# One operand's low part moved to VectorE, PSUM banks handed back singly, and another layout of the last stores, in a fused attention and two-layer kernel

## The chip, the core and the metric

The kernel runs on one core of a Trainium2 chip. Five engines work beside each other, each through its own queue of instructions in order: TensorE (PE, with its weight loads shown as PEld), VectorE (DVE), ScalarE (ACT), GpSimd (POOL) and SyncE (SP), which here only issues DMAs. Engines wait for one another by semaphores. The metric is the time of the kernel on the device, in microseconds (us), median of several runs.

## The reference, cut to what matters

```python
kv = np.einsum('bhsd,bhse->bhde', k, v)            # (4, 8, 64, 64), sum over 576 positions
out = np.einsum('bhsd,bhde->bhse', q, kv)
out = out / np.sqrt(np.mean(out * out, axis=-1, keepdims=True) + 1e-06) * g_norm
x = out.transpose(0, 2, 1, 3).reshape(2304, 512)
h = x @ w_in                                       # layer 1: 512 -> 2048 -> 512
x = (h * (1.0 / (1.0 + np.exp(-h)))) @ w_out
a, b = x @ w_a, x @ w_b                            # layer 2: 512 -> 1536 -> 512
return (a * b) @ w_out2                            # (2304, 512) float32
```

## The kernel before, in words

**Stages.** The 2304 tokens are split into two groups (G = 0 and 1) of 1152, each of two batch rows. After the attention of group 0, the projections run in four segments: layer 1 of group 0, layer 1 of group 1, layer 2 of group 0, layer 2 of group 1 (`SEGS`, numbered 0 to 3, with `PAIR0` = 0, 8, 16, 22, 28). A segment is cut into pairs of 128 hidden columns (8, 8, 6 and 6 of them); the attention of group 1 is done in small pieces between the steps of the first pairs (`attend`, with the steps listed in `KV_AT`, `Q_AT` and so on).

**Products.** Each up projection of a pair is a Strassen scheme of seven products (steps 0 to 6, `step` and `half`, matmuls at L777; L794 for the first two pairs). Every fp32 number is held as a high and a low fp32r part, and each product is made of three: high by high, high by low, low by high. The activations' low parts are `x_lo[:, n]`, one for each of the seven operands, and are made once at the start of a segment: ACT rounds (`x_round`, L1111), then DVE or POOL subtracts (`x_rest`, L1404 for DVE, L634 for POOL). `DVE_RESTS` and `POOL_RESTS` (L87, L88) say which does which, and PE waits for the count that `x_split` gives. In segments 1 to 3 POOL makes the one of operand 6: at the end of `up(u)` (L536 to L558) of the segment's first product. There it stands ahead of the weights of the next product, which POOL also splits (L523, L525).

**Down projections.** The tiles of a pair's down projection are computed one pair later between the steps, by `down1` (L863 to L865, layer 1) and `down2` (L885 to L887, layer 2), in two PSUM banks in turn, BANK_D and BANK_D + 1 (`tile_bank`, from a count of turns). DVE adds each finished tile to `xy` (`flush1` L1473, `flush2` L1484), and `wait_turn` makes PE wait until a bank's last reader is done.

**Keys and values.** `kv(G, h)` (L709) writes both of these banks, and ACT copies the result to `kv_sb` with four copies of 64x64, two for each bank (`kv_keep`, L1077). Both banks are then free at one count, `kv_kept` (L713). For group 1, four such products are made, at the steps in `KV_AT` = (0, 8, 17, 27). Behind the last three stand the rest of a step, of six matmuls, and then a tile of `down1`.

**DVE's queue in layer 2.** The order is written out by hand. In the first pair of segment 2 (`layer2_after_1`, L1608) it is: late_rest 5, flush 3 and 4, `add(ua, 1)`, flush 5. In the other pairs (`layer2`, L1641) it is: late_rest 5, `add(ua, 0)`, flush2 2, `add(ua, 1)`. `add` (L1427) joins two halves of the Strassen sums; PE may begin step 6 only behind `add(ua, 1)` (`may_begin`, L804).

**The end.** After the last pair nine tiles of 128 tokens remain. DVE flushes each, and each is stored by two DMAs, one on SP's queue for the lower 64 partitions and one on ACT's for the upper 64 (`half_tile`; L502, L1310). The ninth is computed and stored in two halves of 256 columns, so as four quarters (`last_down` L899 to L901, `last_flush` L1492, `last_quarter`; L505, L1313). The banks of its halves are those of `last_bank`: the tile's own and the other one of the pair, which tile 8 (j = 7) holds until its flush. The program ends when `stored` has its full count.

Of the kernel before, what the change touches and what calls it, by code (L numbers as in the profile page):

```python
# [15 lines left out]
def fused_attention_ffn_kernel(nc, q, k, v, g_norm, w_in, w_out, w_a, w_b, w_out2, out):  # L16
    BATCH, HEADS, SEQ, HD = q.shape
    D, FF1 = w_in.shape
    FF2 = w_a.shape[1]
    HALF = P // 2  # L20
# [63 lines left out]


    FIRST_ROUNDS = ((0, 0), (7, 0), (0, 1), (7, 1), (3, 0), (6, 0), (3, 1), (6, 1), (5,), (1,), (2,), (4,))
    POOL_RESTS = (((0, 0), (0, 1), (7, 0), (7, 1), (5, 0), (5, 1)), (6,))  # L87
    DVE_RESTS = (((3, 0), (6, 0), (3, 1), (6, 1), (1, 0), (1, 1), (2, 0), (2, 1), (4, 0), (4, 1)),  # L88
                 (0, 1, 2, 3, 4, 5))


    PIECES = [(c, slice(s * PART, (s + 1) * PART)) for c in range(2) for s in range(2)]
# [6 lines left out]
    with ExitStack() as ctx:  # L99
        def sem(name):  # L100
            return ctx.enter_context(nc.semaphore(name))
# [68 lines left out]
        kv_mm = sem("kv_mm")  # L170
        q_ready = sem("q_ready")
        kv_kept = sem("kv_kept")
        kv_kept2 = sem("kv_kept2")
        qT_mm = sem("qT_mm")
        qT_kept = sem("qT_kept")
# [144 lines left out]
            dst = out[(2 * G + m) * SEQ:(2 * G + m + 1) * SEQ].rearrange("(p t) d -> p t d", t=ROWS)[:, n, :]  # L320
            return dst, xy[:, G, :].rearrange("p (j d) -> p j d", d=D)[half * HALF:(half + 1) * HALF, j, :]

        def last_quarter(half, c):

            dst, src = half_tile(GROUPS - 1, TOK_TILES - 1, half)
            cols = slice(c * (D // 2), (c + 1) * (D // 2))
            return dst[:, cols], src[:, cols]

        def staged(G, h):

# [4 lines left out]
            return [(h, j) for h in range(PAIRS) for j in range(JS) if steps[h][j] == at]  # L335


        unit_turn, tile_turn, turns = {}, [], 0
        for pp in range(PAIR0[-1] + 1):
            tiles = D_TILES[SEGS[seg_of(pp - 1)][1]] if pp else 0  # L340
            steps = len(PLAIN[0]) if pp == 1 else STEPS if pp < PAIR0[1] else 0
            for n in range(steps):
                if n < STEPS:
                    at = STEPS * pp + n
                    turns += 2 * KV_AT.count(at)
                    for kind in (RESULT_AT, Q_AT, PROD_AT):
                        for unit in units(at, kind):
                            unit_turn[kind, unit] = turns
                            turns += 1
                for _ in range(0 if pp == 0 else PLAIN_TILES_AFTER[n] if pp == 1 else TILES_AFTER[n]):  # L350
                    tile_turn.append(turns)
                    turns += 1
            for _ in range(tiles if steps == 0 else 0):
                tile_turn.append(turns)
                turns += 1
# [3 lines left out]

        def last_bank(c):  # L360

            return BANK_D + (tile_turn[DOWN0[-1] - 1] + c) % 2

        def unit_bank(kind, h, j):
            return BANK_D + unit_turn[kind, (h, j)] % 2
# [31 lines left out]

        def x_split(seg, n, c=1):

            kind, what = (1, n) if seg else (0, (n, c))  # L400
            if what in POOL_RESTS[kind]:
                at = POOL_RESTS[kind].index(what) + 1
                return side_ready, at + (len(POOL_RESTS[0]) + (seg - 1) * len(POOL_RESTS[1]) if seg else 0)
            at = DVE_RESTS[kind].index(what) + 1
            return x_ready, at + (len(DVE_RESTS[0]) + (seg - 1) * len(DVE_RESTS[1]) if seg else 0)

        def temps(seg):

# [21 lines left out]
        @block.sync  # L430
        def _(sp):
            def raw_free(r):

                n = max(n for n in range(len(SEGS)) if RAW0[n] <= r)
                layer = SEGS[n][1]
                p, what = divmod(r - RAW0[n], layer + 1)
                if what == layer:
                    sp.wait_ge(d_ready, 2 * (PAIR0[n] + p + 1))
                elif p < PLAIN_PAIRS and n == 0:
                    sp.wait_ge(w_ready, RING * (p + 1))  # L440
                else:
                    sp.wait_ge(w_sum, sums_before(PROD0[n] + layer * p + what + 1, 4))

            def load_raw(r):
                n = max(n for n in range(len(SEGS)) if RAW0[n] <= r)
                layer = SEGS[n][1]
                p, what = divmod(r - RAW0[n], layer + 1)
                if r >= RAWS:
                    raw_free(r - RAWS)
                dst = raw[:, r % RAWS, :]  # L450
                cols = slice(2 * p * P, 2 * (p + 1) * P)
                if what == layer:
                    w = w_out if layer == 1 else w_out2
                    dst, src = dst.rearrange("p (f n) -> p f n", f=2), w[cols, :].rearrange("(f p) n -> p f n", p=P)
                else:
                    w = w_in if layer == 1 else (w_a, w_b)[what]
                    dst = dst.rearrange("p (c n) -> p c n", c=KT)
                    src = w.rearrange("(c p) n -> p c n", p=P)[:, :, cols]
                sp.dma_start(dst, src).then_inc(raw_in[r % RAWS], 16)

            def load_heads(h):


                before = PAIRS + h - 1 if h else 0
                sp.wait_ge(kv_mm, before + 1)
                sp.wait_ge(qT_mm, JS * (before + 1))
                for which in range(2):
                    sp.dma_start(*heads(1, h, which)).then_inc(kv_in[0], 16)
                for bb in range(2):
                    for odd in range(2):  # L470
                        sp.dma_start(*head_by_tiles(h, bb, odd)).then_inc(q_in[0], 16)


            for h in range(PAIRS):
                sp.dma_start(*heads(0, h, 0)).then_inc(kv_in[h], 16)
                sp.dma_start(*queries(h, 0)).then_inc(q_in[h], 16)
                if h == 1:
                    for half in range(2):
                        sp.dma_start(gcol[half * HALF:(half + 1) * HALF, 0:1],
                                     g_norm.rearrange("(p a) -> p a", a=1)).then_inc(g_in, 16)  # L480
            sp.dma_start(*raw_half(0)).then_inc(raw_in[0], 16)

            sp.wait_ge(q_in[PAIRS - 1], 32)
            load_heads(0)
            load_raw(1)
            for r in range(2, RAW0[-1]):
                load_raw(r)
                if r == 2:
                    load_heads(1)
                if r == 5:  # L490
                    load_heads(2)
                if r == 8:
                    load_heads(3)
                if r == RAW0[3] + 5:
                    sp.wait_ge(flushed, DOWN0[3])
                    for j in range(TOK_TILES):
                        for half in range(2):
                            sp.dma_start(*half_tile(0, j, half)).then_inc(stored, 16)

            for j in range(TOK_TILES - 1):  # L500
                sp.wait_ge(flushed, down0(PAIR0[-1] - 1) + j + 1)
                sp.dma_start(*half_tile(1, j, 0)).then_inc(stored, 16)  # L502
            for c in range(2):
                sp.wait_ge(flushed, DOWN0[-1] + c)
                sp.dma_start(*last_quarter(0, c)).then_inc(stored, 16)  # L505
            sp.wait_ge(stored, 16 * (2 * GROUPS * TOK_TILES + 2))

        @block.gpsimd
        def _(pool):
# [26 lines left out]
            def up(u):  # L536
# [17 lines left out]
                nc.gpsimd.tensor_tensor(t0, b21, t1, ALU.subtract).then_inc(w_sum, 1)  # L554
                pool.wait_ge(w_sum, done + 4)
                ready(u, 6, t0)
                if u == PROD0[seg_of(pair_of(u))]:
                    x_rest(seg_of(pair_of(u)), 6)  # L558

            def second_up():  # L560

# [125 lines left out]
        def _(pe):  # L687
# [7 lines left out]
            def kv(G, h):  # L695
# [15 lines left out]
                                           start=(t == 0), stop=(t == ROWS - 1))  # L711
                mm.then_inc(kv_mm, 1)
                turn[b0] = turn[b1] = (kv_kept, PAIRS * G + h + 1)  # L713

            def q_turn(G, h, j, bank):
                i = UNITS * G + JS * h + j
# [317 lines left out]
        def _(act):  # L1034
# [30 lines left out]
            def kv_keep(G, h):  # L1065
# [2 lines left out]
                if n >= 2:  # L1068
                    act.wait_ge(o_mm, JS * (n - 1))
                act.wait_ge(cleared, 2)  # L1070
                for odd, bank in enumerate((BANK_D, BANK_D + 1)):
                    if n == 0 and odd:

                        continue
                    rows = slice(odd * HALF, odd * HALF + HD)
                    for bb in range(2):
                        cp = nc.scalar.copy(kv_sb[rows, h % 2, bb, rows], ps[bb * HALF:(bb + 1) * HALF, bank, 0:HD])  # L1077
                cp.then_inc(kv_kept, 1)

            def qT_keep(G, h, j, bank):  # L1080
# [224 lines left out]
                else:  # L1305
                    layer2(pp)
            g_round(PAIR0[-1] - 1, 3)
            for j in range(TOK_TILES - 1):
                act.wait_ge(flushed, down0(PAIR0[-1] - 1) + j + 1)
                nc.scalar.dma_start(*half_tile(1, j, 1)).then_inc(stored, 16)  # L1310
            for c in range(2):
                act.wait_ge(flushed, DOWN0[-1] + c)
                nc.scalar.dma_start(*last_quarter(1, c)).then_inc(stored, 16)  # L1313

        @block.vector
        def _(dve):
# [291 lines left out]
            def layer2_after_1(pp):  # L1608
# [12 lines left out]
                add(ua, 0, halves(held[:, 0, :]))  # L1621
                late_rest(pp, 5)
                flush(3, 4)
                add(ua, 1, halves(held[:, 2, :]))
                flush(5, 5)
                add(ua, 2, halves(held[:, 3, :]))
# [14 lines left out]
            def layer2(pp):  # L1641
# [4 lines left out]
                flush2(pp - 1, 1)  # L1646
                late_rest(pp, 5)
                add(ua, 0, halves(held[:, 0, :]))
                flush2(pp - 1, 2)
                add(ua, 1, halves(held[:, 2, :]))  # L1650
                flush2(pp - 1, 3)
# [83 lines left out]
```

## Time and profile before

| what | value |
|---|---|
| median of 3 runs | 870.26 us (870.24 to 873.62) |
| the profiled execution | 873.04 us, span 871.2 us |
| PE busy | 860.4 us, 99% of the span |
| PEld, DVE, ACT, POOL busy | 93%, 59%, 32%, 70% |
| granted TensorE clock | 0.998 |
| moved by DMA | 55.56 MB, mean 64 GB/s |

The span is what the trace covers, from the first instruction of the program to the last. Times in the trace count from its start. The page lists busy time by engine, the chain of work that ended last, and groups of instructions. In a timeline a row may stand for several equal instructions (x2); its length runs from the first's start to the last's end, and matmuls overlap in their pipeline, so their starts tell more than their lengths. Idle time before an instruction stands in brackets with what ended it.

### The profile page before, as it was taken

Reading aid. Unit: us, or ns where it says so; the run is one execution under the profiler, and the core shown is the slowest. Engines: PE = TensorE matmul, PEld = TensorE weight load, DVE = VectorE, ACT = ScalarE, POOL = GpSimd, SP = SyncE. Lnnn points to the kernel's source line nnn. Section 1 sums busy time; section 2 is a strip of 40 time slices with the busy share of each in tenths; the row PEclk is TensorE's granted clock in tenths of the full one; section 3 lists DMA queues with packets and bytes.
Section 4 is the critical chain, followed back from the end, with each engine's and each line's share of the span. In section 5 each row is a group of like instructions: output and inputs, shape, how many; then the busy total and the mean of one; then the engine's idle time right before and its main releaser. Section 6 shows DMA issues by size and latency. Waiting matters only on the chain.

```text
span 871.2 us, 16097 instructions
## 1 busy us (share of the span) xinstructions
PE 860.4 (99%) x6208; PEld 813.8 (93%) x6208; DVE 510.6 (59%) x776; ACT 279.0 (32%) x465; POOL 610.1 (70%) x889
## 2 busy tenths in 40 slices
PE   8899999999999999999999999999999999999998
PEld 5699999999999999999999999999999999999997
DVE  4665656757886666665765355364484553544636
ACT  3764434534543323222532122121242211212210
POOL 2566545666578777766778697797889876877760
PEclk9999999999999999999999999999999999999999
DMA  9664123111011111111101111021011330210104
GB/s 300 158 156 106 49 57 75 50 49 49 26 49 49 46 28 50 50 49 49 49 25 49 50 49 49 25 63 60 25 49 49 109 98 25 74 49 25 49 25 109
DMA packets 47002, 55.56 MB, mean 64 GB/s; under 512 B 11728, under 2 KB 32464, under 8 KB 46928
## 3 DMA queue, kind: packets, MB, share of 16 engines
q1 hardware_dynamic: 44192, 49.55, 19.9%
q10 hardware_dynamic: 2736, 4.98, 1.8%
q8 instruction: 51, 0.84, 0.4%
q14 instruction: 23, 0.19, 0.1%
HBM read 49.81 MB, written 4.72 MB: 63 GB/s over the span
## 4 chain that ended last, share of the span: by engine, by line
PE 98%; DVE 1%; issue 1%; ACT 0%; POOL 0%; POOLq 0%
PE ps L777 49%; PE ps L863 8%; PE ps L864 8%; PE ps L865 8%; PE ps L885 6%; PE ps L887 6%; PE ps L886 6%; PE ps L794 3%; PE ps L737 2%; PE ps L747 1%; PE ps L989 1%; PE ps L709 1%; PE ps L723 1%; DVE o_sb L1350 0%; DVE stat L1331 0%
## 5 line engine op out<-in xcount | busy, mean ns | idle before, releaser
L777 PE MATMUL ps<-x_hi,w_hi 128*128 128x288 f32 x1064 | 229.8, 297 | 0.5 <-issue 0.3
L777 PE MATMUL ps<-x_lo,w_hi 128*128 128x288 f32 x1064 | 228.1, 296 | 0.0
L777 PE MATMUL ps<-x_hi,w_lo 128*128 128x288 f32 x1064 | 226.8, 295 | 0.0
L777 PEld LDWEIGHTS ps<-x_hi,w_hi 128*128 128x128 f32 x1064 | 179.0, 188 | 13.7 <-issue 5.1
L777 PEld LDWEIGHTS ps<-x_hi,w_lo 128*128 128x128 f32 x1064 | 171.7, 189 | 0.0
L777 PEld LDWEIGHTS ps<-x_lo,w_hi 128*128 128x128 f32 x1064 | 169.9, 188 | 0.0
L1142 ACT COPY kept<-ps 128x576 f32<-128x576 f32 x114 | 73.2, 642 | 288.1 <-PE ps L777 287.6
L523 POOL TENSOR_SCALAR w_hi<-wt 128x256 fp32r<-128x256 f32 x152 | 69.9, 460 | 123.4 <-PE ps L777 116.4
L1473 DVE TENSOR_TENSOR xy<-xy,ps 128x384 f32<-128x384 f32 (+1 forms) x188 | 94.0, 510 | 89.0 <-PE ps L865 88.7
L863 PE MATMUL ps<-g_hi,d_hi 128*128 128x384 f32 x384 | 129.0, 336 | 0.2
L864 PE MATMUL ps<-g_lo,d_hi 128*128 128x384 f32 x384 | 128.9, 336 | 0.0
L865 PE MATMUL ps<-g_hi,d_lo 128*128 128x384 f32 x384 | 128.6, 335 | 0.0
L525 POOL TENSOR_TENSOR w_lo<-wt,w_hi 128x256 fp32r<-128x256 f32 x152 | 114.9, 756 | 12.7
L1484 DVE TENSOR_TENSOR xy<-xy,ps 128x512 f32<-128x512 f32 x89 | 61.0, 685 | 94.2 <-PE ps L887 94.2
L525 POOL TENSOR_TENSOR w_lo<-raw,w_hi 128x256 fp32r<-128x256 f32 x122 | 92.8, 761 | 10.2
L523 POOL TENSOR_SCALAR w_hi<-raw 128x256 fp32r<-128x256 f32 x122 | 52.4, 430 | 57.2 <-PE ps L777 54.2
L885 PE MATMUL ps<-d_hi,g_hi 128*128 128x512 f32 x214 | 84.5, 395 | 0.0
L1167 ACT CAST g_hi<-ps 128x576 fp32r<-128x576 f32 x86 | 55.3, 644 | 89.6 <-DVE ps L1433 54.4
L887 PE MATMUL ps<-d_hi,g_lo 128*128 128x512 f32 x214 | 83.8, 392 | 0.0
L886 PE MATMUL ps<-d_lo,g_hi 128*128 128x512 f32 x214 | 83.6, 391 | 0.0
L1427 DVE TENSOR_TENSOR held<-kept,ps 128x576 f32<-128x576 f32 x62 | 46.8, 755 | 55.6 <-PE ps L777 55.6
L672 POOL TENSOR_TENSOR d_lo<-raw,d_hi 128x512 fp32r<-128x512 f32 x56 | 75.6, 1371 | 0.0
(111 smaller groups left out, 1236.7 us busy)
## 6 DMA issues: line engine op xcount, KB each, us to landing
raw<-in_moe_w_out_dram SPq DMA_DIRECT2D x28, 512.0 KB, 3.6
raw<-in_moe_w_in_dram SPq DMA_DIRECT2D x15, 512.0 KB, 3.5
raw<-in_moe_w_a_dram SPq DMA_DIRECT2D x12, 512.0 KB, 3.5
raw<-in_moe_w_b_dram SPq DMA_DIRECT2D x12, 512.0 KB, 3.5
kvq<-in_k_dram SPq DMA_DIRECT2D x8, 576.0 KB, 5.5
out_dram<-xy SPq DMA_DIRECT2D x26, 128.0 KB, 2.4
kvq<-in_v_dram ACTq DMA_DIRECT2D x4, 576.0 KB, 11.4
kvq<-in_v_dram SPq DMA_DIRECT2D x4, 576.0 KB, 5.9
```

The costliest lines, as they stand in the source:

```text
L523: nc.gpsimd.tensor_scalar(w_hi[:, slot], src, 1.0, 0.0, ALU.mult, ALU.add).then_inc(w_high, 1)
L525: nc.gpsimd.tensor_tensor(w_lo[:, slot], src, w_hi[:, slot].bitcast(F32), ALU.subtract).then_inc(w_ready, 1)
L672: nc.gpsimd.tensor_tensor(d_lo[:, pp % 2, f, :], w[:, f, :], d_hi[:, pp % 2, f, :].bitcast(F32), ALU.subtract).then_inc(d_ready, 1)
L777: mm = pe.matmul(ps[:, bank + s, 0:PART], w, x[:, n, c, s * PART:(s + 1) * PART], start=(begins and first), stop=last, skip_group_check=no ...
L863: pe.matmul(dst, hi, of_high, start=(f == 0), stop=False)
L864: pe.matmul(dst, hi, of_low, start=False, stop=False)
L865: mm = pe.matmul(dst, lo, of_high, start=False, stop=(f == 1))
L885: pe.matmul(dst, hi, d_hi[:, pp % 2, f, :], start=(f == 0), stop=False)
L886: pe.matmul(dst, hi, d_lo[:, pp % 2, f, :], start=False, stop=False)
L887: mm = pe.matmul(dst, lo, d_hi[:, pp % 2, f, :], start=False, stop=(f == 1))
L1142: nc.scalar.copy(halves(kept[:, n, :]), both(BANK_A)).then_inc(part_kept, 1)
L1473: op = nc.vector.tensor_tensor(dst, dst, src, ALU.add)
```

## The change

Four things are changed.

1. The low part of operand 6 in segments 2 and 3 is made by DVE, no more by POOL. In `layer2_after_1` it stands between flush 4 and `add(ua, 1)`, in `layer2` between `add(ua, 0)` and flush2 2. Segment 1 keeps it on POOL.
2. For the keys and values of group 1, a new semaphore `kv_first` is raised after ACT's two copies of the bank whose turn comes first; `kv_order` names it, and `kv_keep` copies it first. The other bank is freed by `kv_kept` as before.
3. The second half of the last tile goes to BANK_A (`last_bank`).
4. The last two tiles are stored over all 128 partitions (`last_tile`): tile j = 7 by one DMA on SP's queue, tile j = 8 by two DMAs of 256 columns each, the first on ACT's queue and the second on SP's. The DRAM side of these is indexed by 2 rows, 64 tokens and the columns; the SBUF side by 128 partitions and the columns.

```diff
-    POOL_RESTS = (((0, 0), (0, 1), (7, 0), (7, 1), (5, 0), (5, 1)), (6,))
+    POOL_RESTS = (((0, 0), (0, 1), (7, 0), (7, 1), (5, 0), (5, 1)), (6,), (), ())
     DVE_RESTS = (((3, 0), (6, 0), (3, 1), (6, 1), (1, 0), (1, 1), (2, 0), (2, 1), (4, 0), (4, 1)),
-                 (0, 1, 2, 3, 4, 5))
+                 (0, 1, 2, 3, 4, 5), (0, 1, 2, 3, 4, 5, 6), (0, 1, 2, 3, 4, 5, 6))
...
-        def last_quarter(half, c):
-
-            dst, src = half_tile(GROUPS - 1, TOK_TILES - 1, half)
-            cols = slice(c * (D // 2), (c + 1) * (D // 2))
-            return dst[:, cols], src[:, cols]
+        def last_tile(j, cols):
+
+
+            n = 2 * j - ROWS
+            dst = out[(2 * GROUPS - 1) * SEQ:].rearrange("(p t) d -> t p d", t=ROWS)[n:n + 2, :, cols]
+            return dst, xy[:, GROUPS - 1, :].rearrange("p (j d) -> p j d", d=D)[:, j, cols]
...
-            return BANK_D + (tile_turn[DOWN0[-1] - 1] + c) % 2
+            return (tile_bank(DOWN0[-1] - 1), BANK_A)[c]
+
+        def kv_order(G, h):
+
+            return (kv_turn[h] % 2, 1 - kv_turn[h] % 2) if G else (0, 1)
...
-            for j in range(TOK_TILES - 1):
+
+            for j in range(TOK_TILES - 2):
                 sp.wait_ge(flushed, down0(PAIR0[-1] - 1) + j + 1)
                 sp.dma_start(*half_tile(1, j, 0)).then_inc(stored, 16)
-            for c in range(2):
-                sp.wait_ge(flushed, DOWN0[-1] + c)
-                sp.dma_start(*last_quarter(0, c)).then_inc(stored, 16)
-            sp.wait_ge(stored, 16 * (2 * GROUPS * TOK_TILES + 2))
+            sp.wait_ge(flushed, DOWN0[-1] - 1)
+            sp.dma_start(*last_tile(TOK_TILES - 2, slice(0, D))).then_inc(stored, 16)
+            sp.wait_ge(flushed, DOWN0[-1] + 1)
+            sp.dma_start(*last_tile(TOK_TILES - 1, slice(D // 2, D))).then_inc(stored, 16)
+            sp.wait_ge(stored, 16 * (2 * TOK_TILES + 2 * (TOK_TILES - 2) + 3))
...
-                if u == PROD0[seg_of(pair_of(u))]:
-                    x_rest(seg_of(pair_of(u)), 6)
+                if u == PROD0[1]:
+                    x_rest(1, 6)
...
                 turn[b0] = turn[b1] = (kv_kept, PAIRS * G + h + 1)
+                if G:
+                    turn[BANK_D + kv_order(G, h)[0]] = (kv_first, h + 1)
...
-                for odd, bank in enumerate((BANK_D, BANK_D + 1)):
+                for place, odd in enumerate(kv_order(G, h)):
...
                     for bb in range(2):
-                        cp = nc.scalar.copy(kv_sb[rows, h % 2, bb, rows], ps[bb * HALF:(bb + 1) * HALF, bank, 0:HD])
+                        cp = nc.scalar.copy(kv_sb[rows, h % 2, bb, rows],
+                                            ps[bb * HALF:(bb + 1) * HALF, BANK_D + odd, 0:HD])
+                    if G and place == 0:
+                        cp.then_inc(kv_first, 1)
                 cp.then_inc(kv_kept, 1)
...
-            for j in range(TOK_TILES - 1):
+            for j in range(TOK_TILES - 2):
                 act.wait_ge(flushed, down0(PAIR0[-1] - 1) + j + 1)
                 nc.scalar.dma_start(*half_tile(1, j, 1)).then_inc(stored, 16)
-            for c in range(2):
-                act.wait_ge(flushed, DOWN0[-1] + c)
-                nc.scalar.dma_start(*last_quarter(1, c)).then_inc(stored, 16)
+            act.wait_ge(flushed, DOWN0[-1])
+            nc.scalar.dma_start(*last_tile(TOK_TILES - 1, slice(0, D // 2))).then_inc(stored, 16)
...
                 flush(3, 4)
+                late_rest(pp, 6)
                 add(ua, 1, halves(held[:, 2, :]))
...
                 add(ua, 0, halves(held[:, 0, :]))
+                late_rest(pp, 6)
                 flush2(pp - 1, 2)
```

## Rows read from the trace of the kernel before

**Rows 1.** The page: busy time by engine, chain that ended last, one group.

```profile
PE 860.4 (99%) x6208; PEld 813.8 (93%) x6208; DVE 510.6 (59%) x776; ACT 279.0 (32%) x465; POOL 610.1 (70%) x889
PE 98%; DVE 1%; issue 1%; ACT 0%; POOL 0%; POOLq 0%
L863 PE MATMUL ps<-g_hi,d_hi 128*128 128x384 f32 x384 | 129.0, 336 | 0.2
```

**Rows 2.** Waits: who waited for what, us in total, times, longest.

```profile
PEld ps L863 <- issue: 0.9, 3, 0.3
PEld ps L777 <- POOL w_lo L525: 0.6, 2, 0.3
PEld ps L899 <- DVE xy L1484: 0.3, 1, 0.3
```

**Rows 3.** Timeline behind the last product of keys: start, length, engine, line, operation.

```profile
143.85 0.87 ACT L1077 COPY kv_sb<-ps 64x64 f32<-64x64 f32 x4 [1.73 <-PE ps L709]
144.34 0.42 PE L777 MATMUL ps<-x_hi,w_lo 128*128 128x288 f32 x2
144.86 0.42 PE L863 MATMUL ps<-g_hi,d_hi 128*128 128x384 f32 x1
```

**Rows 4.** Timeline, PE and POOL, first pair of segment 3.

```profile
658.67 3.10 POOL L637 TENSOR_TENSOR x_lo<-xy,x_hi 128x288 fp32r<-128x288 f32 x4
...
661.21 0.39 PE L887 MATMUL ps<-d_hi,g_lo 128*128 128x512 f32 x1
661.87 0.50 PE L777 MATMUL ps<-x_hi,w_hi 128*128 128x288 f32 x2 [0.27 <-issue]
663.26 0.43 PE L777 MATMUL ps<-x_hi,w_lo 128*128 128x288 f32 x2
663.70 0.53 PE L777 MATMUL ps<-x_hi,w_hi 128*128 128x288 f32 x2
```

**Rows 5.** Timeline, ACT and DVE, the same pair.

```profile
654.62 1.16 ACT L1111 CAST x_hi<-xy 128x1152 fp32r<-128x1152 f32 x1
...
655.69 0.75 DVE L1427 TENSOR_TENSOR held<-kept,ps 128x576 f32<-128x576 f32 x1
658.67 0.69 DVE L1484 TENSOR_TENSOR xy<-xy,ps 128x512 f32<-128x512 f32 x1 [2.23 <-PE ps L887]
```

**Rows 6.** Timeline, DVE and PEld, first pair of segment 2.

```profile
450.79 0.55 DVE L1473 TENSOR_TENSOR xy<-xy,ps 128x384 f32<-128x384 f32 x1 [0.67 <-PE ps L865]
452.39 0.75 DVE L1427 TENSOR_TENSOR held<-kept,ps 128x576 f32<-128x576 f32 x1 [1.04 <-PE ps L777]
...
453.26 0.30 PEld L777 LDWEIGHTS ps<-x_hi,w_hi 128*128 128x128 f32 x2 [0.18 <-issue]
```

**Rows 7.** Line L1406: duration ns min/median/max, first and last start.

```profile
L1406 DVE TENSOR_TENSOR x_lo<-xy,x_hi x6: 1347/1353/1383, 231.3 to 648.9; 128x1152 fp32r<-128x1152 f32 x6
```

**Rows 8.** Timeline of the end, DVE and SP's queue.

```profile
868.18 0.42 DVE L1492 TENSOR_TENSOR xy<-xy,ps 128x256 f32<-128x256 f32 x1 [0.62 <-PE ps L901]
...
857.79 9.82 SPq L502 DMA_DIRECT2D out_dram<-xy  x8
...
867.14 0.47 SPq L502 DMA_DIRECT2D out_dram<-xy  x1
```

**Rows 9.** DMA in 855:872, 855:868 (busy tenths of 40 slices) and 858:868.

```profile
DMA packets 1601, 2.38 MB, mean 140 GB/s; under 512 B 320, under 2 KB 576, under 8 KB 1600
...
DMA  0000000000009993987196909991798378953987
...
q1 hardware_dynamic: 555, 0.91, 43.9%
q10 hardware_dynamic: 550, 0.91, 23.9%
```

**Rows 10.** DMA in 868.5:871.2 (one queue) and 869.4:871.2 (busy tenths).

```profile
q10 hardware_dynamic: 243, 0.27, 30.6%
...
DMA  9986542648999888999783100000000000000000
```

More of the change, by code:

```diff
@@ L172, in fused_attention_ffn_kernel @@
         kv_kept = sem("kv_kept")
+        kv_first = sem("kv_first")
         kv_kept2 = sem("kv_kept2")
@@ L335, in units @@
             return [(h, j) for h in range(PAIRS) for j in range(JS) if steps[h][j] == at]
-        unit_turn, tile_turn, turns = {}, [], 0
+        unit_turn, tile_turn, kv_turn, turns = {}, [], [], 0
         for pp in range(PAIR0[-1] + 1):
@@ L344, in fused_attention_ffn_kernel @@
                     at = STEPS * pp + n
-                    turns += 2 * KV_AT.count(at)
+                    if at in KV_AT:
+                        kv_turn.append(turns)
+                        turns += 2
                     for kind in (RESULT_AT, Q_AT, PROD_AT):
@@ L398, in x_split @@
         def x_split(seg, n, c=1):
[L400 to L405, printed above, removed]
+            what = n if seg else (n, c)
+            split, signal = (POOL_RESTS, side_ready) if what in POOL_RESTS[seg] else (DVE_RESTS, x_ready)
+            return signal, split[seg].index(what) + 1 + sum(len(rests) for rests in split[:seg])
         def temps(seg):
```

## The prediction, made before the changed kernel was built or run

> **What bounds the kernel now.** The page comes first: PE is busy 99% of the span and makes up 98% of the chain that ended last, so only three things can move the time: idle moments of PE, PE's own work (which this change leaves as it is) and what follows PE's last matmul [rows 1]. The list of waits shows how short these moments are: three waits ahead of a `down1` tile (0.9 us in all), two for POOL's weights (0.6), one at the end for a flush (0.3) [rows 2]. Then I read the timeline around each place that the change touches, by the starts of matmuls. In steady work the two matmuls of a kind at L777 start 0.13 apart, so what exceeds this is lost. The end was read from DVE's last flush to the last bytes of the stores. The profiled span is 871.2 us and the median of the runs 870.26; I work out a difference on the span and add it to the median.
>
> **Banks of keys and values.** Behind the last product of keys, the pair of matmuls at 144.34 should be followed by the `down1` tile at 144.34 + 2 x 0.13 = 144.60, and it starts at 144.86, when ACT has made its four copies (143.85 + 0.87 = 144.72) [rows 3]. Lost: 0.26, and another 0.08 because the first matmul after the stop runs 0.42 against a mean of 0.336 [rows 1, 3]. With the bank given back after two copies it is free at about 143.85 + 0.44 = 144.29, before PE wants it. The second bank is wanted a tile later, over 1 us behind, when all four copies are long done. The list of waits has three such stops, of 0.3 each on the load side [rows 2]; the other two lie behind the products at about 61 and 102 us. I take 3 x 0.32 = **-0.97 us** (between -0.7 and -1.0). The fourth product, with other work behind it, has none.
>
> **Operand 6 in segment 3.** POOL's subtraction takes 3.10 us, until 661.77, and PE's step 6 begins at 661.87, where it should have begun at 661.21 + 0.23 = 661.44: 0.43 lost [rows 4]. POOL then comes late with the next product's weights, and PE starts it at 663.70 where 663.26 + 0.26 = 663.52 was due: 0.18 lost, the stop put down to `w_lo` [rows 2, 4]. After the two stops the first pair of matmuls is longer by 0.08 and 0.10 (0.50 and 0.53 against 0.42 to 0.43) [rows 4]. Sum 0.79. On DVE the same subtraction of an operand in `xy` takes 1.35 us in all six cases, never over 1.38 [rows 7]. DVE is free for it: x_hi is there at 655.78, `add(ua, 0)` ends at 656.44, and then DVE idles 2.23 us until the flush at 658.67 [rows 5]. So it is done at 657.8, nothing behind it in DVE's queue moves, and step 6 finds it over 3 us early. Next late there would be `add(ua, 1)`, which has no delay now. I take **-0.80 us**. If the cover of 2.23 us were gone, the flush and PE's bank behind it would come up to 1.35 later.
>
> **Operand 6 in segment 2.** No stop of PE goes here, for POOL's subtraction was early enough. DVE has less room: flush 4 ends at 451.34 and `add(ua, 1)` starts at 452.39, 1.04 us of idle for 1.35 of work [rows 6, 7]. So `add` comes about 0.3 later. PE waits for this very `add` before step 6; its load already idles 0.18 before that [rows 6], so there is no slack and the delay goes to PE in full. **+0.27 us** (from 0.1, if the two operations overlap at their ends, to 0.6, if POOL's traffic slows the subtraction).
>
> **The last bank.** PE stops 0.3 ahead of the last half tile for the flush of tile 8 [rows 2]. BANK_A has been free since the last pair's sums, so the stop goes and the last flush (868.18) comes 0.3 earlier [rows 8]. It counts only if this flush leads to what ends last.
>
> **The last stores.** Here I expect the change to lose. In the last 17 us 20 DMAs leave 320 packets under 512 B, 16 to each: every store so far was shared by 16 DMA engines, which each report once [rows 9]. In all of them both sides have 64 partitions or rows as their outermost dimension. The new ones have 128 partitions on one side, but on the DRAM side an outermost dimension of 2. If a DMA is dealt to the engines along the outermost dimension, only 2 engines can have a share, and each carries 64 rows. No row of before shows such a DMA, so this is bounded from both sides. From below: 16 engines as before, costing nothing. From above: two engines, all three DMAs on the same two. Their speed: in 858:868 one queue moved 0.91 MB in 23.9% of 16 engines' 10 us = 38.2 us, 23.8 GB/s for each busy engine; the other needed 43.9%, so 13.0 GB/s [rows 9]. With rows of 1 KB it was 0.27 MB in 30.6% of 43.2 us = 20.4 GB/s [rows 10]. Tile 8 of the nine is 0.262 MB, 0.131 for each engine: 5.5 us. Tile 9, in rows of 1 KB, as much: 6.4 us. Tile 8's store is issued at 867.14 as before [rows 8]; the first bytes follow an issue by 1.1 us (issue at 857.79, traffic from the thirteenth slice, 858.9) [rows 8, 9]. So the last bytes come at 868.25 + 11.9 = 880.15. Now they come at about 870.4, 0.8 before the end of the span [rows 10]. The end would be at 880.95, **+9.75 us**, and the 0.3 of the last bank isn't on the path.
>
> The Trainium skill, in the page DMA: Bandwidth & Descriptors, section Why a DMA increments its semaphore by 16 and not by 1, says this outright: the number of engines is the largest up to 16 that divides the slowest dimension of both sides, so 2 here, and the lowest-numbered ones. The trace agrees for 64 and 128; no row of it shows a smaller number. The same page speaks for the change in its Rules for kernel authors: two transfers to disjoint halves of the partitions share the same engines, and one over 128 partitions is to be used. By that rule alone the end would be no later than now; that is rival A.
>
> **Sum of the forecast:** -0.97 - 0.80 + 0.27 + 9.75 = +8.25 us on the span, and 870.26 + 8.25 = **878.5 us**.
>
> **Rivals.**
> *All engines share the new stores (A).* Then the last bytes follow the last flush as they do now, with 0.3 from the last bank: -0.97 - 0.80 + 0.27 - 0.3 = -1.8, 868.4 us, no measurable difference. For it: every DMA of the trace has its 16 reports, and the SBUF side still has 128 partitions along which to deal [rows 9]. Against it: both sides must be cut at the same rows, and the DRAM side is offered as 2 blocks of 64. The point of decision is the number of packets under 512 B that the last three stores leave: 48 in this case, about 6 in the forecast. It ends on the other side of the forecast.
> *Two engines at the slower speed (C).* If the two disturb each other as the two queues did, 13.0 GB/s gives 0.262 MB / 13.0 = 20.2 us for each engine, and +18.05 in place of +9.75: 886.8 us. Against it: with two busy engines of 16 there is little to contend for, and most packets should be as fast as the better queue's.
> *The change does not remove the stops (D).* With all engines, but with new waits in the place of the old: a second release on ACT that comes as late as the first, or the 0.27 in segment 2 grown to 1.35 by a flush that is late too. About 870 us, same. Against it are the 0.3 us of room that two copies leave and DVE's 2.23 us of idle [rows 3, 5].
>
> **How the numbers follow.** Forecast 0.63, A 0.25, C 0.05, D 0.05, and 0.02 for A with a gain that I have missed. A measurement of this kernel can tell some 0.5%, 4.35 us, from no change. Slower by more is forecast and C: 0.68. Within it A and D: 0.30. Faster 0.02. The forecast's own range is 876.5 to 881.5: from 23.8 GB/s for both tiles (11.0 us) and first bytes 0.5 sooner, to 18 GB/s for both, midway to the slower queue (14.6 us). As cases on both sides hold most of the chance, the range of 8 in 10 must reach to A: 868.0 to 881.0 us, which leaves out C, the top of the forecast's own range and little else.
>
> **What would show it.** Right: PE's last matmul about 1.8 us earlier than now, near 866; no idle time before the three `down1` tiles; step 6 of segment 3 starting 0.23 behind the matmul before it; in segment 2 a `PEld` idle of about 0.45 in place of 0.18. The last DMAs take over 6 us from issue to landing, DMA is busy at 1 tenth for some 11 us with two engines, and of the packets under 512 B some 230 remain (14 x 16 + 3 x 2). Wrong: the last bytes within 2 us of the last flush, or 272 such packets (17 x 16). If PE ends later than now, the parts on DVE or on ACT were wrong.

## The result and the profile after

The changed kernel took 880.72 us (median of 4 runs, 879.26 to 881.22), the kernel before beside it 870.25 us. The ratio is 1.0106 with a 95% interval of 1.0085 to 1.0127: slower by 7.4 to 11.1 us. The profiled execution took 880.93 us, with a span of 878.9 us.

| | before | after |
|---|---|---|
| median | 870.25 us | 880.72 us |
| span of the profiled execution | 871.2 us | 878.9 us |
| start of PE's last matmul | 867.86 us | 865.49 us |
| from there to the end of the span | 3.4 us | 13.4 us |

The last two rows hold the whole result. PE is done earlier, and what follows it takes four times as long. The page of the changed kernel, busy time by engine and the chain of work that ended last:

```profile
PE 858.8 (98%) x6208; PEld 813.6 (93%) x6208; DVE 513.8 (58%) x778; ACT 278.7 (32%) x465; POOL 605.9 (69%) x881
PE 95%; DMA 2%; DVE 1%; SPq 1%; issue 0%; ACT 0%; POOL 0%
```

PE's busy time fell by 1.6 us against [rows 1]. The 2% of DMA in the chain are not the stores but a load at the start, as the chain in order of time shows (start, length, what):

```profile
5.47 16.00 DMA kvq<-in_q_dram
```

The same 2% stand in the second profile of the kernel before, which has none of the change. This chain ends with DVE's last flush and leaves the stores out, so their price has to be read from the DMA rows.

**The end.** First the timeline of SP's and ACT's queues and of PE in the changed kernel, then its DMA in 867.4:879 (in the two rows of slices each is 0.29 us: busy tenths of the 16 engines, and GB/s), then the DMA packets in 855:879.

```profile
865.10 0.62 SPq L510 DMA_DIRECT2D out_dram<-xy  x1
866.26 0.53 SPq L512 DMA_DIRECT2D out_dram<-xy  x1
...
865.54 1.09 ACTq L1324 DMA_DIRECT2D out_dram<-xy  x1
...
865.49 0.28 PE L910 MATMUL ps<-d_hi,g_lo 128*128 128x256 f32 x1
...
DMA  0020111111111111111111111111111111111000
GB/s 7 35 21 21 35 56 42 56 42 53 56 46 53 49 46 53 49 46 60 42 49 56 46 46 46 49 49 49 49 49 46 46 49 49 49 46 46 7 0 0
...
DMA packets 1511, 2.38 MB, mean 99 GB/s; under 512 B 230, under 2 KB 486, under 8 KB 1510
```

Where [rows 9, 10] have most of the engines busy until 870.4, here one tenth of them (2 of 16) is busy for over 9 us, at 49 GB/s on the mean. The packets under 512 B are 230 = 14 x 16 + 3 x 2: two reports from each of the three new DMAs.

**Behind the keys.** The timeline of the changed kernel behind the last product of keys, as in [rows 3]:

```profile
142.15 0.88 ACT L1086 COPY kv_sb<-ps 64x64 f32<-64x64 f32 x4 [1.73 <-PE ps L716]
142.64 0.43 PE L786 MATMUL ps<-x_hi,w_lo 128*128 128x288 f32 x2
142.91 0.34 PE L872 MATMUL ps<-g_hi,d_hi 128*128 128x384 f32 x1
```

The tile starts at 142.91, 0.27 behind the pair before it, while ACT is still copying the other bank until 143.03. The stop is gone.

**Segment 3.** The end of the tile and the start of step 6, as in [rows 4]; then DVE's new operation with the flush behind it, as in [rows 5]:

```profile
659.92 0.39 PE L896 MATMUL ps<-d_hi,g_lo 128*128 128x512 f32 x1
660.15 0.42 PE L786 MATMUL ps<-x_hi,w_hi 128*128 128x288 f32 x2
...
655.07 1.57 DVE L1417 TENSOR_TENSOR x_lo<-xy,x_hi 128x1152 fp32r<-128x1152 f32 x1
657.38 0.69 DVE L1495 TENSOR_TENSOR xy<-xy,ps 128x512 f32<-128x512 f32 x1 [0.74 <-PE ps L896]
```

Step 6 follows after 0.23, without a stop, and DVE is done 0.74 us before the flush.

**Segment 2.** DVE, POOL and PEld around step 6 of the first pair, as in [rows 6]:

```profile
449.23 1.94 DVE L1417 TENSOR_TENSOR x_lo<-xy,x_hi 128x1152 fp32r<-128x1152 f32 x1
451.09 0.74 DVE L1438 TENSOR_TENSOR held<-kept,ps 128x576 f32<-128x576 f32 x1
...
449.22 0.73 POOL L532 TENSOR_TENSOR w_lo<-wt,w_hi 128x256 fp32r<-128x256 f32 x1
449.92 1.84 POOL L553 TENSOR_TENSOR wt<-raw 128x256 f32<-128x256 f32 x1
...
451.95 0.19 PEld L786 LDWEIGHTS ps<-x_hi,w_hi 128*128 128x128 f32 x1 [0.90 <-issue]
```

The idle time ahead of step 6 grew from 0.18 to 0.90 us. DVE's operation took 1.94 us and not 1.35, and POOL's beside it 1.84, where another of the same shape takes 0.74.

**Step by step on PE.** The same matmul can be found in both traces, since PE's order did not change. How much earlier it starts after the change:

| stretch (times of before) | earlier by | of which here |
|---|---|---|
| until 38 us, ahead of the projections | 1.05 us | 1.05 |
| tiles behind the keys at 64, 104, 145 us | 2.03 | 0.31 + 0.34 + 0.33 |
| step 6 of segment 2, 453 us | 1.29 | -0.74 |
| segment 3, 662 to 664 us | 2.03 | 0.75 |
| last half tile, 867 us | 2.37 | 0.33 |

The first row is not the change, as the second profile of the kernel before shows below. Without it PE is 1.3 us earlier at the end. The gains behind the keys, in segment 3 and at the last bank are read from these starts; they recur in three other kernels with the same parts, but no run takes one of them out alone.

### The profile page after: what moved, and what is told of

Same layout as the page of the kernel before. It is cut to its first block, busy times and chain, and to the rows that moved or that the text cites. A ratio compares the mean times of both kernels' runs of the same rounds, so it can differ in the third digit from the quotient of the medians.

```text
span 878.9 us, 16088 instructions
## 1 busy us (share of the span) xinstructions
PE 858.8 (98%) x6208; PEld 813.6 (93%) x6208; DVE 513.8 (58%) x778; ACT 278.7 (32%) x465; POOL 605.9 (69%) x881
## 4 chain that ended last, share of the span: by engine, by line
PE 95%; DMA 2%; DVE 1%; SPq 1%; issue 0%; ACT 0%; POOL 0%
PE ps L786 48%; PE ps L873 8%; PE ps L874 8%; PE ps L872 8%; PE ps L894 6%; PE ps L896 6%; PE ps L895 6%; PE ps L803 3%; DMA kvq<-in_q_dram 2%; PE ps L746 2%; PE ps L756 1%; PE ps L732 1%; PE ps L716 1%; DVE x_lo L1417 0%; SPq L480 0%
## 5 line engine op out<-in xcount | busy, mean ns | idle before, releaser
L532 POOL TENSOR_TENSOR w_lo<-raw,w_hi 128x256 fp32r<-128x256 f32 x122 | 93.6, 767 | 10.2
```

Of the source, the lines that this page charges most:

```text
L532: nc.gpsimd.tensor_tensor(w_lo[:, slot], src, w_hi[:, slot].bitcast(F32), ALU.subtract).then_inc(w_ready, 1)
```

## The experiments

Each is compared with the kernel before run on the same chip beside it, whose median was 871.5 to 871.7 us there.

### The changed kernel with the old stores

```diff
-            for j in range(TOK_TILES - 2):
+            for j in range(TOK_TILES - 1):
                 sp.wait_ge(flushed, down0(PAIR0[-1] - 1) + j + 1)
                 sp.dma_start(*half_tile(1, j, 0)).then_inc(stored, 16)
...
-            sp.dma_start(*last_tile(TOK_TILES - 2, slice(0, D))).then_inc(stored, 16)
...
+            for c in range(2):
+                sp.wait_ge(flushed, DOWN0[-1] + c)
+                sp.dma_start(*last_quarter(0, c)).then_inc(stored, 16)
...
```

> The changed kernel with the last stores of before (halves and quarters of 64 partitions each), all else as changed. Theory (two engines carry the new stores, and these are the whole loss): the gains that the two profiles show remain, 0.9 us behind the keys, 0.66 in segment 3, 0.3 at the last bank, against 0.64 lost in segment 2, so 1.2 us under the kernel before, about 869.0, with the last bytes within 2 us of the last flush. Rival (part of the loss is elsewhere, since the medians lie 10.5 us apart and the two spans only 7.7): still 0.5 to 3 us above the kernel before, 870.7 to 873.

Measured: ratio 0.9993 (0.9983 to 1.0002), median 870.07 us against 871.52 over 11 runs. The loss is gone with the stores; the rival is ruled out, if narrowly, for it wanted a kernel at least 0.5 us slower than before and the interval ends at +0.2. The ratio is worth 0.6 us, and the expected gain of 1.2 us lies just inside the other edge of the interval. The profile has all the steps of the table at nearly the same sizes (0.31, 0.33, 0.33, -0.70, 0.74, 0.32), but from PE's last matmul to the end it takes 3.7 us, 0.3 more than before. The timeline of this kernel's end shows why: DVE's last flush, and ACT's issue of the last quarter, with that issue in the kernel before behind them:

```profile
866.12 0.42 DVE L1502 TENSOR_TENSOR xy<-xy,ps 128x256 f32<-128x256 f32 x1 [0.30 <-PE ps L908]
...
866.83 0.62 ACTq L1323 DMA_DIRECT2D out_dram<-xy  x1
```

```profile
868.63 0.55 ACTq L1313 DMA_DIRECT2D out_dram<-xy  x1
```

The flush ends at 866.54, and the DMA is issued at 866.83: ACT's queue was still issuing the quarter before. In the kernel before, the issue followed the flush at once (868.60 and 868.63). So what BANK_A gave is taken back by the queue here, where each queue has a DMA for each half tile.

### The new stores alone

```diff
-            for j in range(TOK_TILES - 1):
+            for j in range(TOK_TILES - 2):
...
+            sp.dma_start(*last_tile(TOK_TILES - 2, slice(0, D))).then_inc(stored, 16)
+            sp.wait_ge(flushed, DOWN0[-1] + 1)
+            sp.dma_start(*last_tile(TOK_TILES - 1, slice(D // 2, D))).then_inc(stored, 16)
...
```

> The kernel before with nothing but the new stores of the last two tiles; the order of the banks, of keys and of operand 6 is that of before. Theory: the first bytes 1.1 us behind the issue at 867.1, then 11.3 to 11.9 us on two engines, the end 9.75 us (9.3 to 10.3) later than before, about 880 us, and PE's last matmul where it was. In the DMA rows of the end 230 packets under 512 B. Rival (the loss needs the other parts too, the earlier end of PE or the load of the queues): under +8 us.

Measured: ratio 1.0134 (1.0118 to 1.0149), median 882.21 us. The profile, with SP's issues and its DMA in 855:879.6 (slices of 0.615 us), has the forecast's shape:

```profile
865.75 0.62 SPq L505 DMA_DIRECT2D out_dram<-xy  x1
867.25 0.53 SPq L507 DMA_DIRECT2D out_dram<-xy  x1
...
DMA  0000969678594949596111111111111111111100
GB/s 0 0 0 0 193 233 200 227 153 270 117 270 127 217 150 206 197 203 227 40 20 23 23 43 53 52 50 50 50 50 50 50 48 48 48 48 47 48 33 0
```

From PE's last matmul to the end it takes 13.08 us against 3.39: +9.7, where +9.75 was expected. The interval of the ratio gives 10.3 to 13.0 us, so the timed runs lost at least 0.6 us more than the profiled one. Part of this lies in the start, as the section on the second profile shows: by their mean clock all four runs had the stretch of lower clock there, and the kernel before had it in only 10 of its 21; against these 10 the median lies 10.2 us higher. The rest stays unexplained. The rival (a smaller loss without the other parts) is out.

### One tile, and three tiles, on the new pattern

```diff
-            for j in range(TOK_TILES - 1):
+            for j in range(TOK_TILES - 2):
...
+            sp.wait_ge(flushed, DOWN0[-1] - 1)
+            sp.dma_start(*last_tile(TOK_TILES - 2, slice(0, D))).then_inc(stored, 16)
             for c in range(2):
                 sp.wait_ge(flushed, DOWN0[-1] + c)
                 sp.dma_start(*last_quarter(0, c)).then_inc(stored, 16)
```

> The kernel before, with tile j = 7 alone stored by one DMA over 128 partitions; the last tile in quarters as before. Theory (two engines at 24 GB/s each): 0.131 MB on each engine, 5.4 us from 868.25, with the quarters' rows on the same engines behind or between them: the end 3 to 4.5 us later than before, under half of the loss of both tiles. Rival (a fixed delay for such a DMA, whatever its size): 8 us or more, as with both tiles, or none where the quarters are alone at the end.

Measured: ratio 1.0049 (1.0031 to 1.0066), +2.7 to +5.8 us; in the profile the end lies 8.13 us behind PE's last matmul, +4.7, a little over the expected size. The DMA packets of this kernel in 855:884 are those of 18 plain stores and one on two engines (18 x 16 + 2 = 290):

```profile
DMA packets 1571, 2.38 MB, mean 82 GB/s; under 512 B 290, under 2 KB 546, under 8 KB 1570
```

The rival (a fixed delay of 8 us, or none) is out.

```diff
+            sp.wait_ge(flushed, DOWN0[-1] - 2)
+            sp.dma_start(*last_tile(TOK_TILES - 3, slice(0, D))).then_inc(stored, 16)
+            sp.wait_ge(flushed, DOWN0[-1] - 1)
+            sp.dma_start(*last_tile(TOK_TILES - 2, slice(0, D))).then_inc(stored, 16)
...
```

> The kernel before with three tiles (j = 6, 7 and 8) stored as the changed kernel stores two. Theory (all such DMAs queue on the same two engines, and their bytes set the end): one more tile of 0.262 MB is 5.5 us on the two engines, of which 1.36 us lie ahead of the issue of the next: the end 4.0 to 4.5 us later than with two tiles, some 14 us later than before, near 884.5 us. Rival (each DMA has two engines of its own): no later than with two tiles.

Measured: ratio 1.0146 (1.0127 to 1.0164), median 884.37 us. From PE's last matmul to the end it takes 17.0 us, 3.9 more than with two tiles and 13.6 more than before. The DMA of this kernel in 855:884 (slices of 0.725 us):

```profile
GB/s 0 82 268 170 204 178 198 201 178 229 172 226 76 37 42 23 34 45 51 54 51 51 45 51 51 51 51 51 51 51 48 51 48 48 49 49 14 0 0 0
DMA packets 1481, 2.38 MB, mean 82 GB/s; under 512 B 200, under 2 KB 456, under 8 KB 1480
```

Four such DMAs share the same 49 to 51 GB/s and leave 12 x 16 + 4 x 2 = 200 small packets. The loss thus goes by bytes (4.7, 9.7 and 13.6 us for one, two and three tiles), it is no fixed delay, and the DMAs don't get two engines each, which would give 98 GB/s.

### Rows that two divides and four does not

```diff
+        def rows_of(j, half):
+            dst, src = half_tile(1, j, half)
+            cut = 62 if j == TOK_TILES - 2 else HALF
+            return [(dst[a:b], src[a:b]) for a, b in ((0, cut), (cut, HALF)) if a < b]
...
-                sp.dma_start(*half_tile(1, j, 0)).then_inc(stored, 16)
+                for dst, src in rows_of(j, 0):
+                    sp.dma_start(dst, src).then_inc(stored, 16)
```

> The kernel before, with the two halves of tile j = 7 each stored as 62 partitions and then the last 2, so plain patterns of 62 x 512 and 2 x 512 on both sides. Theory (a DMA is shared by the largest number of engines up to 16 that divides the outermost counts): 2 engines for each of the four, 64 rows of 2 KB on each of the same two engines, 5.4 us, and the last quarters behind them: the end 3 to 4.5 us later than before, and 296 packets under 512 B in the last 17 us in place of 320. Rival (only the outermost dimension of 2 in the DRAM pattern confines it, plain rows are spread over all): at most 0.5 us later, and over 320 such packets.

Measured: ratio 1.0072 (1.0054 to 1.0091). The DMA packets in 855:884, and SP's queue:

```profile
DMA packets 1577, 2.38 MB, mean 82 GB/s; under 512 B 296, under 2 KB 552, under 8 KB 1576
...
867.77 2.54 SPq L512 DMA_DIRECT2D out_dram<-xy  x2
```

There are 296 small packets (18 x 16 + 4 x 2): the 62 rows of a plain pattern went to two engines as well. So it is a divisor of the outermost counts that decides, and not the form of the pattern with its block of 2. The Trainium skill states this rule in the page DMA: Bandwidth & Descriptors, section Why a DMA increments its semaphore by 16 and not by 1; the 230, 290, 200 and 296 packets agree with it. The runs have only the cases of 2 and 16 engines, so they can't tell the largest divisor up to 16 from the largest power of two.

The size was missed: from PE's last matmul to the end it takes 9.8 us, +6.4 where 3 to 4.5 was expected. The issue of the last two quarters on SP's queue took 2.54 us. The same two issues in the kernel before, and in the kernel with one tile on the new pattern:

```profile
867.65 1.44 SPq L505 DMA_DIRECT2D out_dram<-xy  x2
```

```profile
866.49 1.30 SPq L514 DMA_DIRECT2D out_dram<-xy  x2
```

With one tile on the new pattern two engines were loaded too, yet the issue was no longer than before. So a load on two engines is not enough to hold the issuing queue back; here both queues feed them, and each has one more DMA to issue. The two engines moved some 0.29 MB (the tile and their share of the quarters) between about 868.1 and 876.5, which is an estimate of 35 GB/s for both, against 49 before. Why this is slower wasn't settled.

### POOL held while DVE subtracts

```diff
                 if u == PROD0[1]:
                     x_rest(1, 6)
+                if u == PROD0[2]:
+                    pool.wait_ge(*x_split(2, 6))
```

> The changed kernel, with POOL held in the first pair of segment 2 until DVE has made the low part of operand 6. In the changed kernel this DVE operation took 1.94 us beside POOL's work, against 1.35 in six cases of the kernel before. Theory (DVE and POOL slow each other down where both work in SBUF): 1.35 to 1.40 us, and the stop ahead of step 6 falls from 0.78 to about 0.2 us. Rival (DVE is slowed by something else there, such as the traffic of a load, or the place in the queue): 1.9 us and 0.7 to 0.8 as before.

DVE's and PEld's timeline of this kernel, and POOL's wait:

```profile
450.27 1.35 DVE L1419 TENSOR_TENSOR x_lo<-xy,x_hi 128x1152 fp32r<-128x1152 f32 x1
...
452.40 0.30 PEld L788 LDWEIGHTS ps<-x_hi,w_hi 128*128 128x128 f32 x2 [0.32 <-issue]
...
451.70 0.74 POOL L547 TENSOR_TENSOR wt<-raw 128x256 f32<-128x256 f32 x1 [5.78 <-DVE x_lo L1419]
```

DVE takes 1.35 us again. By the starts of matmuls PE loses 0.20 us before step 6, as expected, where it lost 0.78 in the changed kernel and 0.06 in the kernel before. So POOL's work beside it had made the operation slow. The one run took 881.34 us and says nothing about the gain: the lower clock at its start lasted 6.8 us, twice as long as in the changed kernel.

The timeline of the changed kernel, above, fits turns taken: DVE starts at 449.23, just behind POOL's operation of 0.73 at 449.22, and 0.7 + 1.35 is about its 1.94; POOL's next, begun at 449.92, ends 0.6 behind DVE's. The Trainium skill describes this in the page SBUF — State Buffer, section SBUF: two separate sides: a DVE operation with two SBUF inputs and a GpSimd one that reads SBUF need the same pair of ports, and whichever starts first holds it for its whole length. The rows agree within 0.2 us.

The trace of the kernel before had already shown it, in the groups of the same line that [rows 7] leaves out:

```profile
L1406 DVE TENSOR_TENSOR x_lo<-kvq,x_hi x9: 1346/1550/2443, 234.9 to 651.5; 128x1152 fp32r<-128x1152 f32 x9
L1406 DVE TENSOR_TENSOR x_lo<-qT_sb,x_hi x2: 1785/1836/1887, 447.8 to 653.8; 128x1152 fp32r<-128x1152 f32 x2
L1406 DVE TENSOR_TENSOR x_lo<-held,x_hi x1: 1942/1942/1942, 258.8 to 258.8; 128x1152 fp32r<-128x1152 f32 x1
```

The shape is the same, and only the input differs. The one of 1.94 us starts 0.08 us behind an operation of POOL, as in the changed kernel. When the six of `xy` started, no operation of POOL had more than 0.2 us left; where one began in their first 0.6 us, POOL's was the one that grew (to 1.72 us, at 649.18).

### Operand 6 of segment 2 back on POOL

```diff
-    POOL_RESTS = (((0, 0), (0, 1), (7, 0), (7, 1), (5, 0), (5, 1)), (6,), (), ())
+    POOL_RESTS = (((0, 0), (0, 1), (7, 0), (7, 1), (5, 0), (5, 1)), (6,), (6,), ())
...
                 flush(3, 4)
-                late_rest(pp, 6)
```

> The changed kernel with the stores of before and with operand 6 of segment 2 back on POOL; the keys' banks, operand 6 of segment 3 on DVE and BANK_A stay. Theory: the stop of 0.78 us ahead of step 6 in segment 2 shrinks to the 0.05 of before, so 0.7 us less than with DVE, about 868.3, 0.2% under the kernel before. Rival (that stop is caused by something else that moved, such as PE being earlier): it stays at 0.5 or more.

Measured, with the old stores as in the first experiment: ratio 0.9985 (0.9973 to 0.9997), median 870.37 us against 871.52. PEld ahead of step 6 in segment 2 idles as before:

```profile
451.52 0.30 PEld L784 LDWEIGHTS ps<-x_hi,w_hi 128*128 128x128 f32 x2 [0.18 <-issue]
```

The 0.7 us is back: by the starts of matmuls no more is lost here than in the kernel before, and PE's last matmul starts at 865.08. From there to the end it takes 3.9 us, 0.5 more than before: the last flush ends at 865.82 and ACT issues the last quarter only at 866.19, as in the first experiment. The kernel is 0.15% under the kernel before, with an interval that just excludes no change. The medians of this kernel and of the first experiment (870.37 and 870.07) don't tell the two apart; the traces do, and so do runs with a like start, as the next section shows.

### The kernel before, profiled again

> The kernel before, unchanged, profiled once more. The profiled execution of before took 873.04 us where three others took 870.2, so its span is long by 2.8 us. Theory: the difference lies in the first 35 us, where the inputs come in and PE waits, and from 40 us on the two profiles run alike within 0.2 us. Rival: the difference lies in the end, and the price of the new stores read from the profiles is then too small by it.

It took 871.89 us, with a span of 870.1 us. The first matmuls of the projections in the kernel before, in this second profile, and in the changed kernel:

```profile
38.49 0.53 PE L794 MATMUL ps<-x_hi,w_hi 128*128 128x288 f32 x2
```

```profile
37.31 0.52 PE L794 MATMUL ps<-x_hi,w_hi 128*128 128x288 f32 x2
```

```profile
37.44 0.53 PE L803 MATMUL ps<-x_hi,w_hi 128*128 128x288 f32 x2
```

Between two profiles of one kernel the start alone differs by 1.2 us; from there on they agree within 0.1 us, and at the end both take 3.4 us from PE's last matmul. So the rival is out: the price of the stores was read rightly from the end, and the 1.05 us at the head of the table belongs to no part of the change.

There is a second difference in the start that these two profiles don't show, for both have it. For 3.4 us the granted TensorE clock is at 0.5, its lower level of 1.2 GHz. In the kernel before it begins at 27.5 us, 0.4 us after PE had ended 2.3 us of idle time. The stretch in the kernel before, and the same moment in the kernel with three tiles, which kept the full 2.4 GHz (the third number from the end is the clock):

```profile
27.60:30.90 3.30, 3.30 (x22) 2.16 (x18) 0.69 (x2) 1.56 (x3) 2.98 (x5) 0.50 0.95 326
```

```profile
26.60:29.90 3.30, 3.30 (x78) 2.57 (x78) 1.15 (x3) 2.59 (x5) 2.41 (x5) 1.00 0.49 146
```

The kernel with 62 rows also kept the full clock there, though its PE had idled 2.3 us at the same place, so that idle time alone doesn't decide.

The mean clock of each run beside the experiments tells which of the two starts it had. Of the 28 runs of the kernel before, 13 have 1.000 and took 869.9 to 871.1 us, one has 0.999 and took 871.6, and 14 have 0.997 or 0.998 and took 871.5 to 874.5. So a median depends on how many runs had the one start or the other. Compared within each group, the changed kernel with the old stores lies 1.0 us under the kernel before at 0.999 and more (medians of 6 runs against 11) and 0.5 us at the lower clock (5 against 10). With operand 6 of segment 2 back on POOL it lies 2.2 us under it (2 against 11) and 1.6 us (9 against 10). These groups are small, but in both the second kernel is the lower one by more than 1 us, where the traces give it 0.7 us on PE.

## Why the prediction was right, step by step

The forecast was 878.5 us in a range of 868.0 to 881.0, slower with a chance of 0.68; 880.72 lies in the range, near its top.

- **Stores:** right in mechanism, and right in size with some luck. Forecast were 230 small packets, one tenth of the engines busy, and 13.8 us from the issue of tile j = 7 (867.14) to the end (880.95). Measured are 230, one tenth, and 865.10 to 878.9, 13.8 us. Rival A (all engines share) is ruled out by the packets, rival C (13.0 GB/s) by the 49 GB/s of both engines together. But two errors cancel in the 13.8. For rows of 1 KB the forecast took 20.4 GB/s for each engine, and both kinds of rows went at 24 to 25, which saves about 1 us. And the first DMA started at half speed, for which the forecast had no term: the DMA of the changed kernel in 866:879 (slices of 0.325 us) has 19 to 32 GB/s from about 866.7 to 868.9, which costs about as much.

```profile
GB/s 32 50 19 25 25 25 25 32 32 50 50 50 50 47 50 57 44 50 50 50 50 50 47 54 47 50 44 50 50 44 50 50 44 50 47 47 50 19 0 0
```

- **Keys' banks:** forecast -0.97, measured -0.98.
- **Segment 3:** forecast -0.80, measured -0.75. DVE needed 1.57 us and had room.
- **Segment 2:** forecast +0.27 with a range from 0.1 to 0.6, measured +0.74; the load's idle time was to be 0.45 and was 0.90. This is the term that was mis-sized. The step that failed is the price of 1.35 us "in all six cases": none of the six had been slowed by POOL, while twelve others of the same line and shape took 1.35 to 2.44 us. Moving the work off POOL brought POOL's next operations to just this moment. With POOL held, the cost is 0.14 us (0.20 against the 0.06 of before), inside that range.
- **Last bank:** forecast -0.3, off the path; measured -0.33, off the path. Rival A had counted it as a gain, and there it would have failed: with the old stores the issue of the last quarters takes it back.
- **PE's last matmul:** forecast 1.8 us earlier, measured 1.3 without the start (2.37 - 1.05); what is missing is segment 2.
- **Rival D** was half right in segment 2 alone: a new wait in place of none.
- **Range:** from the two speeds that it names, the forecast's own range comes out as 877.1 to 881.2, not 876.5 to 881.5.
- **The sum** by the traces: -0.98 + 0.74 - 0.75 = -0.99 on PE, and from the issue of the store of tile j = 7 to the end 13.8 us in place of 4.1 (867.14 to 871.2), +9.7. Together +8.7 us, inside the interval of 7.4 to 11.1. That the median lies at +10.5 has to do with the start. Three of the four runs of the changed kernel have a mean clock of 0.993, like its profile, which has the lower clock at the start and again behind PE's last work; the fourth has 0.995, which fits the second stretch alone, and took 879.26 us. That is 9.0 us over the three runs of the kernel before at 870.2. The clocks of those three are not on record, but in the other series every run of the kernel before under 871.1 us had the full clock. So the forecast was nearer than 880.72 against 878.5 suggests, and that the time came so near to the top of the range is in good part the start's doing.

## What to carry to other kernels

Before two DMAs are merged into one over more partitions, look at the outermost count of both sides: 64 rows went to 16 engines, while 62 rows, and 2 blocks of 64, went to 2. A block of 2 on the DRAM side cost 4.7 us for one tile at the end, far more than a saved issue gave. The number of tiny packets in the DMA rows tells at once how many engines took part. When work is moved from POOL to DVE, look at what POOL will then do at that moment, and read the price from all rows of that shape and not from those with the same input alone. Where a part is worth under 1 us, compare matmul starts of the two traces rather than medians, and look at the granted clock of each run before comparing medians.

## What the runs showed of the hardware beyond this

- A DMA confined to two engines moved 48 to 51 GB/s, and several of them, from SP's and ACT's queues, shared that rate.
- DMAs from both queues to the same two engines, with 62 rows each, moved some 35 GB/s (an estimate), and the issue of the next two DMAs took 2.54 us in place of 1.44. The cause stays open.
- The first DMA on two engines moved 19 to 32 GB/s for its first 2 us, then about 50.
- An elementwise operation of DVE with both inputs in SBUF took 1.35 us with POOL held and 1.94 just behind the start of one of POOL's, and POOL's next took 1.84 in place of 0.74.
- In the start of the kernel the granted clock fell to its lower level for 3.4 us in some executions and not in others; the runs of one kernel split by it into 869.9 to 871.1 us and 871.5 to 874.5 us.
